# The last tile of a routed MLP taken out of the expert loop, and the tile counts moved ahead

## What is computed

```python
kv  = einsum('bhsd,bhse->bhde', k, v)          # (8, 8, 576, 64) inputs
o   = einsum('bhsd,bhde->bhse', q, kv)
x   = o / rms(o) * g_norm                      # as 4608 tokens x 512
x   = square(relu(x @ w_in)) @ w_out           # 512 -> 2048 -> 512
logits = x @ w_gate + modality_bias[modality_id]
e   = argmax(logits)                           # one of 8 experts for a token
gate = softmax(logits)[e]
out[tokens of e] = gate * (relu(x @ w1[e]) @ w2[e])   # 512 -> 1024 -> 512
```

## Time and profile before

| | |
|---|---|
| time, median of 3 runs | 1445.43 us (1442.05 to 1445.94) |
| time of the profiled execution | 1443.15 us |
| its span | 1441.4 us, 26597 instructions |
| PE busy | 1398.4 us, 97% |
| DVE busy | 827.2 us, 57% |
| ACT busy | 615.6 us, 43% |
| POOL busy | 500.3 us, 35% |
| mean granted clock of TensorE | 0.987 |

### The profile page before, as it was taken

How to read it: one execution, slowest core, us unless ns; L and a number is a source line. 1 busy time by engine, 2 the same in 40 slices (tenths; PEclk the granted TensorE clock), 3 DMA queues, 4 the chain that set the end, 5 groups by cost and what they waited for, 6 DMA issues and landing times.

```text
span 1441.4 us, 26597 instructions
## 1 busy us (share of the span) xinstructions
PE 1398.4 (97%) x8257; PEld 1276.0 (89%) x8257; DVE 827.2 (57%) x1875; ACT 615.6 (43%) x1306; POOL 500.3 (35%) x593
## 2 busy tenths in 40 slices
PE   5899999999999999999999999999999999999997
PEld 4799999999999999999999999987778887888785
DVE  3365656565665747565656566455655555555553
ACT  2354333333433433333333333235555555555553
POOL 2452313121222222222312122432555555555552
PEclk8999999999999999999999999998999999999999
DMA  7642766665566667376666465697696112751260
GB/s 166 169 121 92 175 158 201 131 201 118 183 148 185 151 191 154 134 164 177 189 141 198 98 190 118 225 243 244 246 367 229 45 45 100 301 202 47 90 233 24
DMA packets 210301, 237.64 MB, mean 165 GB/s; under 512 B 95517, under 2 KB 128701, under 8 KB 210178
## 3 DMA queue, kind: packets, MB, share of 16 engines
q1 hardware_dynamic: 200578, 215.90, 52.5%
q0 software_dynamic: 9600, 20.22, 4.2%
HBM read 148.33 MB, written 88.77 MB: 164 GB/s over the span
## 4 chain that ended last, share of the span: by engine, by line
PE 90%; DMA 4%; DVE 2%; issue 1%; SPq 1%; POOL 1%; ACT 1%; POOLq 0%; DVEq 0%; ACTq 0%
PE ps_h L995 15%; PE ps_y L995 15%; PE ps_h L808 9%; PE ps_h L810 9%; PE ps_h L809 9%; PE ps_y L810 9%; PE ps_y L808 8%; PE ps_y L809 8%; PE ps_a L846 2%; PE ps_b L876 1%; DMA stage<-in_moe_w_in 1%; DMA stage<-in_moe_w 1%; DMA w_lo<-stage 1%; PE ps_a L876 1%; PE ps_a L860 1%
## 5 line engine op out<-in xcount | busy, mean ns | idle before, releaser
L663 POOL TENSOR_TENSOR stage<-stage,stage_hi 128x512 f32<-128x512 f32 x128 | 169.7, 1326 | 605.4 <-ACT stage_hi L1131 605.1
L1455 DVE TENSOR_TENSOR g_sb<-relu_sb 128x384 f32<-128x384 f32 x192 | 117.5, 612 | 293.7 <-ACT relu_sb L1189 275.8
L1189 ACT ACTIVATE relu_sb<-ps_h 128x384 f32<-128x384 f32 x192 | 94.2, 490 | 435.4 <-PE ps_h L810 418.7
L808 PE MATMUL ps_h<-xT_hi,weights 128*128 128x384 f32 x768 | 267.7, 349 | 7.3 <-POOL weights L655 3.5
L808 PE MATMUL ps_y<-g_hi,weights 128*128 128x384 f32 x768 | 261.6, 341 | 2.4 <-issue 1.5
L809 PE MATMUL ps_h<-xT_lo,weights 128*128 128x384 f32 x768 | 258.6, 337 | 0.0
L810 PE MATMUL ps_h<-xT_hi,weights 128*128 128x384 f32 x768 | 258.5, 337 | 0.0
L810 PE MATMUL ps_y<-g_hi,weights 128*128 128x384 f32 x768 | 257.2, 335 | 0.0
L809 PE MATMUL ps_y<-g_lo,weights 128*128 128x384 f32 x768 | 256.8, 334 | 0.0
L1217 ACT ACTIVATE kv_sb<-ps_h 32x256 f32<-32x256 f32 x468 | 175.2, 374 | 127.9 <-PE ps_h L995 122.3
L736 POOL DMA_INDIRECT k_sb<-rows,idx x152 | 150.9, 993 | 89.2 <-issue 48.3
(11 more groups left out here) (229 smaller groups left out, 1774.4 us busy)
## 6 DMA issues: line engine op xcount, KB each, us to landing
stage<-in_moe_w SPq DMA_DIRECT2D x128, 256.0 KB
w_hi<-stage_hi SPq DMA_DIRECT2D x128, 256.0 KB
w_lo<-stage SPq DMA_DIRECT2D x128, 256.0 KB
weights<-w_hi SPq DMA_DIRECT2D x32, 1024.0 KB
weights<-w_lo SPq DMA_DIRECT2D x32, 1024.0 KB, 6.5
rows<-y_sb SPq DMA_DIRECT2D x48, 192.0 KB
k_sb<-in_k SPq DMA_DIRECT2D x60, 144.0 KB, 3.5
v_sb<-in_v SPq DMA_DIRECT2D x30, 288.0 KB, 4.1
```

Of the source, the lines that this page charges most:

```text
L663: pool.tensor_tensor(stage[n % 2][:, :], stage[n % 2][:, :], stage_hi[n % 2][:, :].bitcast(F32), ALU.subtract).then_inc(piece_lo, 1)
L808: pe.matmul(out_ap, lhs[0], rhs[0], start=start, stop=False)
L1189: act.activation(relu_sb[:, :], ps_h[c % 2][:, 0:GROUP], ACT.Relu).then_inc(h_read, 1)
L1455: dve.tensor_tensor(g_sb[:, :], relu_sb[:, :], relu_sb[:, :], ALU.mult).then_inc(g_done, 1)
```

## The change

The last tile is taken out of every engine's loop. The last expert's number of tiles gets a floor of 3 and is then lowered by one, so that its loop ends one tile sooner. Behind the loop each engine has its own code for the last tile. `penult` is the tile before it.

TensorE signals each half of the last hidden products by itself (`half_hidden`). ScalarE and VectorE move each half with 8 blocks of 32 by 128 each (instead of 12 and 4 blocks of 32 by 256). VectorE then turns both halves and makes the low parts ahead of the copy of the output before. The parts go to `last_h`, which lies in `xT[2]`, the output goes to bank `ps_y[3]`, is copied to `last_rows` (the buffer into which rows are fetched) and sent with ids from `last_idx`. Rows beyond the last tile are no longer fetched, turned and split.

Apart from that, `count_tiles` and `keep_early` stand ahead of `next_ids` and the move of tile 1 on VectorE.

```diff
+LEAST_LAST = 3
+        def half_to_move(a, b, half):
+            return ps_hidden[a * QUAD:(a + 1) * QUAD, half * 512:(half + 1) * 512].rearrange("p (k b x) -> p k b x", k=4, b=4)[:, :, b, :]
+        def half_move_to(a, b, half):
+            return h_moved[b * QUAD:(b + 1) * QUAD, half, a, :].rearrange("p (k x) -> p k x", k=4)
+        last_h = [xT[2][s][:, :, :].rearrange("p k t -> p (k t)")[:, 0:FC * P].rearrange("p (f t) -> p f t", f=FC)
+                  for s in range(2)]
+        LAST_MOVES, LAST_OWN_MOVES = ([(a, b) for a in range(4) for b in range(4)][x] for x in (slice(0, 8), slice(8, 16)))
+        last_rows, last_idx = fetch_to, idx[:, 0:1]
...
@@ GpSimd, behind the loops
-            last = last_tile(pool)
-            for half in range(2):
-                pool.wait_ge(rows_turned[half], last + 1)
-                fetch(last + 1, idx, (half,))
-            scatter(last, -2)
-            scatter(last, -1)
-            pool.wait_ge(out_sent, last * 16)
-            pool.tensor_copy(out_idx[:, :], tile_ids[:, bass.ds(last, 1)]).then_inc(out_idx_set, 1)
-            pool.wait_ge(out_idx_set, last + EARLY)
-            pool.wait_ge(y_by_dve, last + (GROUPS + 1))
-            send_rows()
+            penult = one_before_last(pool)
+            tile(penult, E - 1, tiles_of(pool, E - 1))
+            scatter(penult, -1)
+            pool.wait_ge(rows_turned[0], penult + 2)
+            pool.wait_ge(rows_turned[1], penult + 2)
+            pool.tensor_copy(last_idx, tile_ids[:, bass.ds(penult + 1, 1)]).then_inc(idx_set, 1)
+            scatter(penult, 0)
+            pool.wait_ge(idx_set, penult * 2 + 3)
+            pool.wait_ge(y_by_dve, penult + (GROUPS + 2))
+            pool.indirect_dma_start(out, bass.IndirectOffsetOnAxis(ap=last_idx, axis=0), last_rows, None,
+                                    bounds_check=N - 1, oob_is_err=False).then_inc(out_sent, 16)
...
@@ TensorE, behind the loops
-            output_of(last_tile(pe), (E - 1) % 2)
+            penult, n = one_before_last(pe), (E - 1) % 2
+            pe.wait_ge(x_lo_done, penult + (ROWS + 2))
+            pe.wait_ge(relu_done, penult + 1)
+            pe.wait_ge(own_moves_done, penult + 1)
+            hidden(penult + 1, n, 0, 0, 3 * KC, half_hidden)
+            hidden(penult + 1, n, 1, 0, 3 * KC, half_hidden)
+            output_of(penult, n)
+            pe.wait_ge(hT_lo_done, penult * 2 + 3)
+            output(n, 0, 12, ps_y[3], last_h)
+            pe.wait_ge(hT_lo_done, penult * 2 + 4)
+            output(n, 12, 3 * FC, ps_y[3], last_h)
...
@@ ScalarE, behind the loops
+            penult = one_before_last(act)
+            act.wait_ge(hT_done, penult * 2 + 2)
+            for half in range(2):
+                act.wait_ge(half_hidden, half + 1)
+                for a, b in LAST_MOVES:
+                    last = act.activation(half_move_to(a, b, half), half_to_move(a, b, half), ACT.Relu)
+                last.then_inc(relu_done, 1)
+            for half in range(2):
+                act.wait_ge(hT_done, penult * 2 + (half + 3))
+                act.activation(in_quarters(last_h[0][:, 4 * half:4 * half + 4, :]), by_chunk(h_turned[half]), ACT.Copy).then_inc(hT_hi_done, 1)
...
@@ VectorE, count_tiles
                 then(dve.tensor_scalar(tiles_i[0:1, 0, 1:E], tiles_i[0:1, 1, 1:E], LEAST, None, ALU.max))
+                then(dve.tensor_scalar(tiles_i[0:1, 0, E - 1:E], tiles_i[0:1, 0, E - 1:E], LEAST_LAST, None, ALU.max))
                 then(dve.tensor_copy(counts[0:1, 0, :], tiles_i[0:1, 0, :]))
+                then(dve.tensor_scalar(tiles_i[0:1, 0, E - 1:E], tiles_i[0:1, 0, E - 1:E], -1, None, ALU.add))
@@ VectorE, the list before the loops
             h_lo(0, 1)
+            count_tiles()
+            keep_early()
             next_ids()
             move_h(1)
-            count_tiles()
-            keep_early()
             turn_h(1, 0)
@@ VectorE, behind the loops
-            copy_out(last_tile(dve))
+            penult = one_before_last(dve)
+            dve.wait_ge(hT_done, penult * 2 + 2)
+            for half in range(2):
+                dve.wait_ge(half_hidden, half + 1)
+                for a, b in LAST_OWN_MOVES:
+                    last = dve.tensor_scalar(half_move_to(a, b, half), half_to_move(a, b, half), 0.0, None, ALU.max)
+                last.then_inc(own_moves_done, 1)
+            for half in range(2):
+                dve.wait_ge(relu_done, penult + (half + 2))
+                dve.wait_ge(own_moves_done, penult + (half + 2))
+                dve.wait_ge(hT_lo_done, penult * 2 + 2)
+                dve.transpose(h_turned[half], h_moved[:, half, :, :].rearrange("p a r -> p (a r)")).then_inc(hT_done, 1)
+            for half in range(2):
+                dve.wait_ge(hT_hi_done, penult * 2 + (half + 3))
+                hi, lo = (in_quarters(last_h[s][:, 4 * half:4 * half + 4, :]) for s in range(2))
+                dve.tensor_tensor(lo, by_chunk(h_turned[half]), hi.bitcast(F32), ALU.subtract).then_inc(hT_lo_done, 1)
+            copy_out(penult)
+            dve.wait_ge(y_ps, penult + (GROUPS + 2))
+            dve.tensor_copy(last_rows, ps_y[3][:, :]).then_inc(y_by_dve, 1)
```

More of the change, by code:

```diff
@@ L313, in routed_mlp_program @@
             sem(x) for x in ("own_moves_done", "early_kept", "ids_kept"))
-        kept_in, slots_done, slot_ids_ps, ids_in_block_done, next_ps, next_set, ids_ready = (
-            sem(x) for x in ("kept_in", "slots_done", "slot_ids_ps", "ids_in_block_done", "next_ps", "next_set", "ids_ready"))
+        kept_in, slots_done, slot_ids_ps, ids_in_block_done, next_ps, next_set, ids_ready, half_hidden = (
+            sem(x) for x in ("kept_in", "slots_done", "slot_ids_ps", "ids_in_block_done", "next_ps", "next_set", "ids_ready", "half_hidden"))
         idx_set, out_idx_set, scaled, early_to_in = (
@@ L377, in tiles_of @@
         def tiles_of(eng, e):
-            return eng.value_load(tiles_i[0:1, 0, e:e + 1], min_val=LEAST if e else 1, max_val=LIST // P)
+            return eng.value_load(tiles_i[0:1, 0, e:e + 1], min_val=LEAST if e else 1, max_val=LIST // P - (e == E - 1))
         def tile_before(eng, e):
@@ L392, in all_experts, with one_before_last @@
                     at_tile(previous + t, e, t)
-        def last_tile(eng):
+        def one_before_last(eng):
             return tiles_of(eng, E - 1) + tile_before(eng, E - 1)
@@ L784, in _ @@
             all_experts(pool, tile, first_ids)
-            last = last_tile(pool)
-            for half in range(2):
-                pool.wait_ge(rows_turned[half], last + 1)
-                pool.sem_inc(passed, 1)
-                fetch(last + 1, idx, (half,))
-            scatter(last, -2)
-            scatter(last, -1)
-            pool.wait_ge(out_sent, last * 16)
+            penult = one_before_last(pool)
+            tile(penult, E - 1, tiles_of(pool, E - 1))
+            scatter(penult, -1)
+            pool.wait_ge(rows_turned[0], penult + 2)
             pool.sem_inc(passed, 1)
-            pool.tensor_copy(out_idx[:, :], tile_ids[:, bass.ds(last, 1)]).then_inc(out_idx_set, 1)
-            pool.wait_ge(out_idx_set, last + EARLY)
+            pool.wait_ge(rows_turned[1], penult + 2)
             pool.sem_inc(passed, 1)
-            pool.wait_ge(y_by_dve, last + (GROUPS + 1))
+            pool.tensor_copy(last_idx, tile_ids[:, bass.ds(penult + 1, 1)]).then_inc(idx_set, 1)
+            scatter(penult, 0)
+            pool.wait_ge(idx_set, penult * 2 + 3)
             pool.sem_inc(passed, 1)
-            send_rows()
-            pool.wait_ge(out_sent, last * 16 + 16)
+            pool.wait_ge(y_by_dve, penult + (GROUPS + 2))
+            pool.sem_inc(passed, 1)
+            pool.indirect_dma_start(out, bass.IndirectOffsetOnAxis(ap=last_idx, axis=0), last_rows, None,
+                                    bounds_check=N - 1, oob_is_err=False).then_inc(out_sent, 16)
+            pool.wait_ge(out_sent, penult * 16 + 32)
             pool.sem_inc(passed, 1)
@@ L997, in products, with hidden, output @@
                 return last
-            def hidden(T, n, half, a, b):
+            def hidden(T, n, half, a, b, signal=None):
                 last = products(hidden_bank(T)[:, half * 512:(half + 1) * 512], x_B(T),
                                 [w1_B[n][s][:, :, half * 512:(half + 1) * 512] for s in range(2)], KC, a, b)
-                if b == 3 * KC:
+                if signal is not None:
+                    last.then_inc(signal, 1)
+                elif b == 3 * KC:
                     last.then_inc(h_ps, 1)
-            def output(n, a, b):
-                last = products(ps_y[0][:, :], h_B, w2_B[n], FC, a, b)
+            def output(n, a, b, out_bank=ps_y[0], h=h_B):
+                last = products(out_bank[:, :], h, w2_B[n], FC, a, b)
                 if b == 3 * FC:
```

## The result

| | before | changed |
|---|---|---|
| median of the runs in which both were timed | 1442.53 us (8 runs, 1439.44 to 1445.94) | 1435.64 us (8 runs, 1434.39 to 1436.17) |
| profiled execution | 1443.15 us, span 1441.4 | 1434.79 us, span 1433.0 |
| sends of rows to `out` | 40 | 39 from L761 and 1 from L810 |

The ratio is 0.9949 with a 95% interval of 0.9937 to 0.9961: 7.4 us less (5.6 to 9.1), where 7.1 were forecast. The medians of the table lie 6.9 apart. The time named was 1437.2 us, and 1435.64 came: most of the 1.6 between them is the starting point, since the median of before that I had, 1445.43 of three runs, is 1442.53 over eight. The number of tiles is the same.

A forecast was written before the change was run, and what follows sets the result against it. TensorE was taken as the bound, with gains only at its waits before tile 3's hidden products (2.6 us) and the last output (4.5 us): 7.1 us, between 1436.05 and 1438.3, named 1437.2 us, range 1433.3 to 1441.8.

The forecast's parts named there:

- Row stores as the gate: Before tile 3: GpSimd's first table copy waits for the row stores, taken to land at 992.7, so it comes 1.7 us earlier.
- place one: TensorE's wait of 3.15 us before tile 3's hidden products, and the slow clock in them; forecast gain 2.6 us.
- rival of early stores: Before tile 3: row stores in by 990.9, gain there 5.6 us, whole 10.1, time 1434.2 us; chance 0.06.
- The counts: VectorE's tile counts, started ahead of the ids and the move of tile 1, are there at 989.36, 3.67 us earlier.
- The fetch keeps its 5.35 us: Tile 3's fourth row fetch still takes 5.35 us from issue to VectorE, since the weight traffic beside it does not move.
- The idle time of 1.45 us: TensorE's idling before tile 3's hidden products shrinks to 1.45 us from 3.15.
- sign of being wrong: The prediction is wrong if either gap, before tile 3's or the last output's products, stays at 3 us.
- The clock falls at the cheaper price: At tile 3's hidden products TensorE's clock still falls after the idling, costing 1.88 us (bounds 0 and 2.77).
- Half moves 0.30 us: Last tile's h: each 32x128 move on VectorE takes 0.30 us with its gap, 16 of them 4.8 us.
- 0.3 us left open: Before the last output's products TensorE waits only about 0.3 us and the clock stays up; gain at the end 4.5 us.
- The sum: Whole kernel: 2.6 us before tile 3 plus 4.5 at the last tile, 7.1 us gained; time named 1437.2 us.
- An empty tile: Last expert's loop: the floor of three adds an empty tile of 11.15 us, net +4.05, time 1448.4 us; chance 0.04.

The follow-up runs named there:

- rows-first: Changed kernel, but SyncE loads the second half of expert 1's weights only once tile 3's rows have landed: 1437.33 us, ratio 0.9974 to before.
- The end alone: Changed kernel with the old order of the counts, so only the last tile is taken out of the loop: 1438.02 us, ratio 0.9977 to before.
- counts only: Kernel before with only the counts and early ids moved ahead of the ids and the move of tile 1: 1440.41 us, ratio 0.9992 to before.
- copy first: Changed kernel, but VectorE copies the output before ahead of the last tile's turns again: 1441.69 us, ratio 1.0004 to before.

## Why the prediction was right, step by step

- **Row stores as the gate.** This was the choice on which place one hung: the landing was not in the trace, I took it as that of the id sends beside it. It held: 1.77 us earlier against 1.7, and the releaser is named. Of this 0.40 was lost in GpSimd's slower copies and 0.27 won back in the fetch, neither of which was forecast. Every profile of the new order has it, 10.0 to 11.0 us behind the slot product. The estimate of 3.4, by the section of the Trainium skill that the prediction names ("DMA: Bandwidth & Descriptors", Anatomy of one DMA), was off; that section is about DMAs issued by GpSimd, and these stores are issued by SyncE. The rival of early stores is refuted.
- **The counts** end 4.3 us earlier counted from the slot product, against 3.67. Most of the rest is TensorE's clock at the slot products, for which VectorE waited 0.88 us before and 0.36 now. It had no effect, since the stores end later.
- **The fetch keeps its 5.35 us.** It took 5.08. The rows-first kernel shows that about 2.4 of it are the weight traffic.
- **The idle time of 1.45 us** was wrong: 4.55. I took TensorE's arrival as fixed; the clock did not fall at the slot products, and TensorE came 3 us earlier to a gate that does not depend on it. The start of tile 3's products was right nonetheless (1.64 earlier against 1.7), since the fetches set it. So the prediction's sign of being wrong, a gap that stays at 3 us, appeared (4.55) although the gain was there: the length of a gap does not tell what was won before it.
- **The clock falls at the cheaper price.** It fell, 24 products and the step to the output took 7.16 us, 1.45 more than the usual 5.71, against 1.88. Sum at place one 2.8 against 2.6. In timed runs this part alone is worth 1.2 us with zero inside the interval: one profile of before, in which the clock had fallen at the slot products, made it look surer than it is. Without that fall the old order would be at the gate just in time. An estimate from the two profiles: in the changed one the product for the ids ends at 984.96. Before, the end of the counts lay 4.61 us behind that product (988.42 to 993.03), which makes 989.57, and with 1.53 for the loads GpSimd would be ready at 991.10, where the stores release it at 991.15. I had not weighed that case. That the 2.6 us agree with the profiles is luck to that extent.
- **Half moves 0.30 us.** They took 0.305, on ScalarE 0.284. The line through two forms held. The 0.258 of the Trainium skill's table ("VectorE: DVE Perf Modes", the section on the TRN2 errata) was too low, as its 0.392 for 256 columns was beside 0.428 here. Its rule that many small tiles pay the fixed cost each time agrees with what was seen: 16 half moves took VectorE 4.88 us, 8 whole ones 3.5.
- **0.3 us left open** at the end: it was 0.52, because the loop exit took 1.08 instead of 0.91 and the 16 moves 4.88 instead of 4.8; the chain of turn, high part and low part took 2.15, where 2.2 was reckoned. And behind such a gap the last 24 products took 5.76 us, not 5.45. Together 4.12 instead of 4.5.
- **The sum.** The end alone timed at 3.3 us (1.6 to 4.9) where 4.5 were forecast, place one at 1.2 (0.7 more to 3.0 less) where 2.6 were, the whole at 7.4 and 5.9. All intervals hold the forecast, but three of the four values lie under it. The profiled pair agrees better than the times do because the clock of before had fallen at both places in it. And no term of the sum stood for the stretch behind place one, in which three other profiles (counts only, copy first, rows first) lose 2 to 4 us.
- **An empty tile**: none, 40 sends.

## What to carry to other kernels

Where a tail stands open, look first at what an in-order engine does ahead of the work that the tail needs: here moving one copy behind the turns was the gain of the end, and own buffers were, by the code, the price of being allowed to; the cut into halves added nothing. A chain that starts with bookkeeping should not stand behind a wait for the busy engine, even if a profile shows the bookkeeping as cheap: its worth shows in the executions in which that engine is late. And a gain in one place is a gain of the kernel only if the stretch behind keeps its length: here a transfer moved out of one fetch's way landed in the next one's.

## What the runs showed of the hardware

- The same products ran at a granted clock of 0.50 in one execution and 1.00 in another (985 to 991 us in the profiles before and after), and a gap of 2.9 us before the last output was followed by a fall of the clock in one and not in the other. One profile can't price such a gap: here it was 2.4 or 4.1 us. Before tile 3, 2.2 us of idling were followed by 1.00 in one kernel and 2.4 us by 0.68 in another.
- The row stores, 768 KB, were signalled at 991.15, about 4 us after the DMA traffic had ended (nothing from 987 to 991 in the changed kernel's window); before, the traffic was at 0.28 until 989.0 and the load of the lists, which waits for the sends of ids, stood until 992.71. From the issue of the fourth row fetch to its turn it took 4.3 to 5.9 us in the twelve profiles with the weights beside it, and 2.7 in the rows-first kernel.
- A move of 32x128 out of PSUM costs 0.305 us on VectorE, one of 32x256 0.43: by these two some 0.18 us of each (an estimate) do not depend on the columns, so a cut into halves has to save more than it repeats.
